# Value products and transposes on alternate steps: TensorE transposes two tiles in a row at even steps and does two or three blocks of the value product at odd steps

## The reference

```python
scores = q @ k.T / sqrt(64)
thresh = max(scores, axis=-1) - tau
scores = where(scores >= thresh, scores, -1e9)
attn   = exp(scores - max) / (sum + 1e-9)
x      = attn @ v                      # reshaped to 2304 x 512
h = x @ w_in;  x = (h - tanh(h)) @ w_out        # 512 -> 2048 -> 512
h = x @ w_in2; x = (h * sigmoid(h)) @ w_out2    # 512 -> 2048 -> 512
```

## Time and profile before

| | before |
|---|---|
| median of 3 runs | 1010.98 us |
| the profiled execution's own time | 1011.08 us |
| its span | 1009.2 us |
| PE busy | 990.1 us (98%) |
| DVE busy | 828.9 us (82%) |
| ACT busy | 716.6 us (71%) |
| POOL busy | 463.3 us (46%) |

### The profile page before, as it was taken

One profiled execution on the slowest core, in us unless ns is written; L12 is line 12 of the kernel. 1 busy time (PEld: TensorE's weight loads), 2 busy tenths in 40 slices (PEclk: granted clock), 3 DMA queues, 4 the chain that ended last, 5 costly groups with the idle time before them and its releaser, 6 DMA issues.

```text
span 1009.2 us, 18094 instructions
## 1 busy us (share of the span) xinstructions
PE 990.1 (98%) x6002; PEld 900.3 (89%) x6002; DVE 828.9 (82%) x1633; ACT 716.6 (71%) x1441; POOL 463.3 (46%) x509
## 2 busy tenths in 40 slices
PE   6999999999999999999999999999999999999998
PEld 5666767676669999999999999999999999999998
DVE  8999999999988999698996989776895559935675
ACT  6999999999977766477646767387664676457642
POOL 5999999999977420164104540074201340024000
PEclk9999999999999999999999999999999999999999
DMA  6254453625213867438772577538785257724286
GB/s 213 79 179 156 168 200 127 242 92 184 88 38 123 275 219 251 152 111 274 231 257 89 187 245 245 179 105 275 222 251 170 64 188 232 249 105 168 77 254 211
DMA packets 57867, 181.00 MB, mean 179 GB/s; under 512 B 5040, under 2 KB 6576, under 8 KB 57776
## 3 DMA queue, kind: packets, MB, share of 16 engines
q1 hardware_dynamic: 57488, 179.78, 54.3%
q10 hardware_dynamic: 288, 0.07, 0.0%
HBM read 145.75 MB, written 34.08 MB: 178 GB/s over the span
## 4 chain that ended last, share of the span: by engine, by line
PE 90%; DVE 5%; issue 2%; ACT 1%; POOL 0%; ACTq 0%; DVEq 0%
PE b L1313 32%; PE b L1395 32%; PE scores L1274 10%; PE pv L1237 10%; PE tps L1296 7%; DVE g_op L1134 1%; DVE x_sum L1068 1%; DVE c L1120 1%; DVE c L1103 1%; DVE b L1088 0%; DVE w_op L1045 0%; ACT b L840 0%; DVE stage L1053 0%; DVE probs L1009 0%; DVE probs L977 0%
## 5 line engine op out<-in xcount | busy, mean ns | idle before, releaser
L1313 PE MATMUL b<-x_op,w_op 128*128 128x384 f32 x2016 | 354.1, 335 | 1.0 <-ACT b L840 0.8
L1395 PE MATMUL b<-g_op,w 128*128 128x384 f32 x2016 | 352.6, 334 | 0.6 <-DVE g_op L1134 0.5
L1313 PEld LDWEIGHTS b<-x_op,w_op 128*128 128x128 f32 x2016 | 349.0, 188 | 4.2 <-ACT b L840 3.1
L1395 PEld LDWEIGHTS b<-g_op,w 128*128 128x128 f32 x2016 | 349.4, 188 | 2.0 <-issue 2.0
L568 POOL TENSOR_TENSOR w_sum<-w_raw 128x256 f32<-128x256 f32 x94 | 74.7, 795 | 254.7 <-PE b L1313 254.0
L977 DVE TENSOR_SCALAR_CACHE_REDUCE probs<-scores,fine 128x576 f32<-128x576 f32 x144 | 116.9, 811 | 12.2 <-PE scores L1274 11.5
L882 ACT ACTIVATE g_op<-c 128x768 fp32r<-128x768 f32 x96 | 81.2, 846 | 61.0 <-DVE c L1120 34.1
L1274 PEld LDWEIGHTS scores<-k_lo,q_parts 128*128 128x128 f32 x336 | 64.0, 193 | 64.9 <-issue 38.3
L1045 DVE TENSOR_TENSOR w_op<-w_sum,w_op 128x512 fp32r<-128x512 f32 x94 | 76.1, 810 | 54.6 <-ACT w_op L795 54.3
L644 POOL TENSOR_SCALAR probs<-probs,rinv 128x576 f32<-128x576 f32 x144 | 109.7, 762 | 18.7 <-DVE rinv L1002 11.6
L1009 DVE SCALAR_TENSOR_TENSOR probs<-scores,stats,probs 128x576 f32<-128x576 f32 x144 | 117.8, 818 | 0.1
(11 more groups left out here) (89 smaller groups left out, 1340.6 us busy)
## 6 DMA issues: line engine op xcount, KB each, us to landing
w<-scr SPq DMA_DIRECT2D x168, 512.0 KB, 4.5
w_raw<-w_in SPq DMA_DIRECT2D x56, 512.0 KB, 3.8
scr<-w_op SPq DMA_DIRECT2D x8, 1792.0 KB, 8.3
scr<-stage SPq DMA_DIRECT2D x8, 1792.0 KB, 9.0
k_raw<-k_in SPq DMA_DIRECT2D x15, 576.0 KB, 5.9
q_raw<-q_in SPq DMA_DIRECT2D x15, 576.0 KB, 7.1
v_all<-v_in SPq DMA_DIRECT2D x16, 320.0 KB, 3.2
stage_raw<-w_in SPq DMA_DIRECT2D x8, 512.0 KB, 4.0
```

The costliest lines, as they stand in the source:

```text
L1313: last = pe.matmul(out, a, b, start=fresh and k == 0 and i == 0, stop=k == 1 and i == 2, skip_group_check=True)
L1395: last = pe.matmul(bank[n][kind], x, y, start=fresh and q == 0 and f == 0 and i == 0, stop=q == 3 and f == 1 and i == 2, skip_group_check= ...
```

## The change

PE transposes nothing at odd steps. At even steps it transposes the tiles of k - 14 and k - 13, one behind the other. The value product comes at odd steps alone. With two lists (`L_PV[0]` for pairs 0 and 2 of a batch, `L_PV[1]` for pairs 1 and 3) a pair has four value steps (2, 3, 2, 3 blocks) or five (2, 2, 1, 2, 3 blocks). For pairs 0 and 2 ACT copies a finished half one step earlier than before. ACT still takes one step's transposes in each of its steps, but at odd steps it does so behind the exponential and no longer ahead of it. The scores, DVE and POOL keep their lists.

```diff
-L_PV = {L_T + 8: (0, 0, 1), L_T + 9: (0, 1, 2), L_T + 10: (0, 2, 3), L_T + 11: (0, 3, 5),
-        L_T + 12: (1, 0, 1), L_T + 13: (1, 1, 2), L_T + 14: (1, 2, 3), L_T + 15: (1, 3, 5)}
-L_OUT = {L_T + 12: 0, L_T + 16: 1}
-TAIL = (PAIRS - 1) * TILES + max(L_OUT) + 1
+L_PV = ({L_T + 8: (0, 0, 2), L_T + 10: (0, 2, 5), L_T + 12: (1, 0, 2), L_T + 14: (1, 2, 5)},
+        {L_T + 7: (0, 0, 2), L_T + 9: (0, 2, 4), L_T + 11: (0, 4, 5), L_T + 13: (1, 0, 2), L_T + 15: (1, 2, 5)})
+L_OUT = {L_T + 11: 0, L_T + 15: 1}, {L_T + 12: 0, L_T + 16: 1}
+TAIL = (PAIRS - 1) * TILES + max(L_OUT[1]) + 1
...
+                for k in ks:
+
+                    for parity, lag, a in ((i, *item) for i in range(2) for item in L_OUT[i].items()):
+                        q = k - lag
+                        if q % TILES == 0 and q // TILES % 2 == parity and here(q):
...
+                    if k % 2 == 0:
+                        take_transposes(k)
+                    exponential(k)
+                    if k % 2 == 1:
+                        take_transposes(k)
...
-                    for lag, (a, i0, i1) in L_PV.items():
+                    for parity, lag, (a, i0, i1) in ((i, *item) for i in range(2) for item in L_PV[i].items()):
                         q = k - lag
-                        if q % TILES == 0 and here(q):
+                        if q % TILES == 0 and q // TILES % 2 == parity and here(q):
...
+                for k in ks:
+                    scores_of(k)
+                    if k % 2 == 0:
+                        transposes_of(k - 1)
+                        transposes_of(k)
                     product(k)
```

More of the change, by code:

```diff
@@ L715, in here, with take_transposes @@
                     return q < STEPS and (q >= 0 or not first)
-                for k in ks:
-                    for lag, a in L_OUT.items():
-                        q = k - lag
-                        if q % TILES == 0 and here(q):
[L722 to L726, removed]
+                def take_transposes(k):
                     for kind, q, number in units_of(k - L_T, first):
@@ L744, in steps, with exponential @@
                         last.then_inc(t_taken, 1)
+                def exponential(k):
                     q = k - L_EXP
@@ L751, in steps @@
                                        accum_out=rowsum[:, c:c + 1]).then_inc(exp_done, 1)
+                for k in ks:
+                    for parity, lag, a in ((i, *item) for i in range(2) for item in L_OUT[i].items()):
+                        q = k - lag
+                        if q % TILES == 0 and q // TILES % 2 == parity and here(q):
+                            p, i = q // TILES, 2 * (PAIRS * B + q // TILES) + a
+                            act.wait_ge(pv_done, i + 1)
+                            for to, of in columns(B + p // PAIRS, a):
+                                last = act.activation(xT[:, p % PAIRS, to], pv[:, of], ACT.Copy)
+                            last.then_inc(out_taken, 1)
+                    if k % 2 == 0:
[3 more added lines that the diff above has]
+                        take_transposes(k)
                     if k < STEPS:
@@ L1240, in product, with scores_of @@
                                 last.then_inc(pv_done, 1)
-                for k in ks:
+                def scores_of(k):
                     q = k - L_S
@@ L1276, in steps, with transposes_of @@
                         last.then_inc(scores_done, 1)
+                def transposes_of(k):
                     for kind, q, number in units_of(k - L_T, first):
```

## The result

| | before | changed |
|---|---|---|
| median | 1011.0 us (6 runs, 1010.93 to 1011.94) | 1015.05 us (6 runs, 1013.85 to 1015.38) |
| the profiled execution's own time | 1011.08 us | 1013.88 us |
| its span | 1009.2 us | 1012.0 us |

The changed kernel is slower: ratio 1.0036, 95% interval 1.0026 to 1.0046. The forecast was 1013.9 us, in a range of 1009.5 to 1017.8. The runs of the changed kernel come in two groups, two at 1013.9 us with a mean granted clock of 1.000, the profiled one like them, and four at 1015.0 to 1015.4 us with 0.998. All that the profiles show belongs to the first group, where the change costs 2.8 us.

A forecast was written before the change was run, and what follows sets the result against it. TensorE at 17.56 us a pair and GpSimd at 17.6 were taken as equally full. Lateness of 2.0 us by the last scaling plus 0.9 in the tail, on 1011.08, gave 1013.9 us, range 1009.5 to 1017.8.

The forecast's parts named there:

- ScalarE's 1 us: ScalarE's work over one pair before the change: 16.5 us, 6% below the pace.
- PE's sum: TensorE's work for 18 steps, two pairs: 32.6 us after the change, 35.1 before, from fewer switches.
- direct switch from scores: TensorE going from scores straight to a value product at odd steps: taken as 0.16 us, bounded by 0.20.
- The 20 us: TensorE's saving over 16 pairs from fewer switches if it alone set the time, giving 991 us.
- The loop: Lateness passing from ScalarE through VectorE and TensorE back to ScalarE: 0.3 us in two pairs, 2.0 by the last scaling.
- Waits of VectorE for exponentials: VectorE waiting for late exponentials: 2.5 us over 18 steps, in six or seven steps, up to 1.1 us each.
- Value products waiting: TensorE's value products waiting for their bank: 1.85 us over 18 steps; 20 places or more, 10 us or more in all.
- the layout: Four engine queues laid side by side from trace durations: 35.8 us for 18 steps, against 35.5 before.
- waits for masks: TensorE's scores waiting for VectorE's masks: 1.4 us over 18 steps.
- The tail: Behind the last scaling: two bank waits of 1.5 us, fewer switches and one block less, 0.9 us more in all.
- waits for roundings: GpSimd waiting for ScalarE's roundings: 3.5 us more, beside the other waits and not on top.
- A: Rival: no difference, ScalarE's 6% to spare absorbs the lateness and GpSimd sets the time; 1010.5 to 1011.5 us, chance 0.30.

The follow-up runs named there:

- the half scaling: The kernel before with GpSimd scaling only 288 of each tile's 576 columns: 1010.51 us, ratio 0.9992.
- their combination: The kernel before with value products as in the changed kernel, one transpose group a step, and GpSimd scaling only half of each tile: 1000.27 us, ratio 0.9891.
- copies_last: The changed kernel with ScalarE taking the transposes at the very end of its step at odd steps: 1009.78 us, ratio 0.9986.
- products_only: The kernel before with the changed kernel's value products at odd steps, still one transpose group in every step: 1009.60 us, ratio 0.9984.
- products_short_dve: The kernel before with the changed kernel's value products, and each weight block's fourth piece moved from GpSimd to VectorE: 1005.77 us, ratio 0.9945.

## Why the prediction was right

**What bounds the kernel before.** PE and GpSimd are both full: shown by the half scaling, the product steps and their combination (-0.7, -1.6, -11 us). VectorE is next: 0.9 us a pair behind by the prediction's sum, 0.7 as measured (17.0 us a pair in that combination, 17.7 before). ScalarE's 1 us is a sum that no run tests.

**PE's sum.** 16 switches became 9 in two pairs at 0.36 us. The direct switch from scores, not to be seen before, was taken as 0.16 and is 0.17 (1.61 - 3 x 0.48). The Trainium skill ("TensorEngine Tiling (Array Packing)", Key Properties) says that changing the tiling mode drains TensorE. A price of 0.17 us at that switch agrees with it, though no run shows that a drain is what costs it. The 20 us that fewer switches alone would give did not come, as the loads of the other engines said.

**The loop.** 35.8 us for 18 steps were laid out, 0.3 more than before; 35.60 were measured on average, 0.23 more. Waits of VectorE for exponentials: 2.5 us in 18 steps expected, 16.1 in all measured over some 14.6 pairs, so 2.2. Value products waiting: 20 times, 8.8 us, where I had said 10 or more; that is 1.2 us in 18 steps, where the layout had 1.85. TensorE's listed waits for masks are 6.1 us, 0.8 in 18 steps, where it had 1.4; some of the rest may be hidden in scores that take 0.68 and 0.75 us in the chain (at 240.84 and 212.91) where 0.52 is the price without a wait. At the last scaling +2.06 us (2.0 forecast). That the total comes so close, with its parts off by a third, is in part luck: the prediction itself had the layout at +1.2 to +5.6 for a switch cheaper or dearer by 0.1 to 0.16 us.

**The tail.** 0.9 us forecast, 0.81 measured, and the same in `copies_last` against `products_only` (10.43 and 9.61 us). The two waits were 1.33 and 1.25 us, not 1.5 each.

**GpSimd.** Its waits for roundings rose by 2.9 us, to 3.7 (3.5 more forecast), and, as said, beside the others: half the scaling changes nothing.

**What was missed.** The median is 1.2 us above the profiled execution: the group of runs at the lower clock was not foreseen, and forecast and profile agree better (2.9 and 2.8 us) than forecast and median (2.9 and 4.05). Among the rivals, A (ScalarE's slack absorbs it) was wrong by the order of a queue: with the copies at the end of the step it does absorb it, but for the tail. And the split of the loss between the product bank and the row sum, both of which the layout has, stays open.

## What to carry to other kernels

When several engines are full to a per cent, add up what one period costs each of them before paying for a cheaper one: 20 us less work for TensorE bought 1.6 us while GpSimd was full, and 10.2 once it was not (1010.51 to 1000.27). Work moved from one to another of two engines that get in each other's way costs both. When a producer starts to deliver in pairs, look at the consumer's in-order queue, and ask of each instruction behind the copy who waits for it; put the copy that can wait last. Laying the queues side by side from the trace's own durations gave the time of every reordering here to 3 us; the one miss of more was a duration that changed on another engine. The single waits it gave less well.

## What the runs showed of the hardware

A subtraction on VectorE with both inputs in SBUF and an operation of GpSimd did not run side by side. The same subtraction of 128x512 took VectorE 0.68 to 1.58 us, and GpSimd's of 128x576 took 1.85 us beside it instead of 1.42. The short one of 128x256 took 0.42 to 1.29 us in `products_short_dve`, 0.80 on average. The last scaling of the kernel before is of this kind too. It starts at 291.36, inside the first of VectorE's two subtractions of 128x768 (lines 1080 and 1076, from 291.07 to 292.90), and takes 2.07 us instead of 0.75.

Switching TensorE from 128-column scores to 64-column products costs 0.17 us, as it does from transposes. The changed kernel ran with a mean granted clock of 0.998 and 1.2 us more time in 7 of 11 executions, while two kernels with the same two waits in the tail did so in none of 18.
